# Six explicit drains of GpSimd in a fused attention, MLP and routed-expert kernel: one beside the MLP, one in each unrolled block of the expert loop

## The chip, the cores and the metric

The kernel runs on one core of one Trainium2 chip. The metric is the device time of one execution in microseconds (us), lower is better. It is given as the median of several executions. Engines are named as the profile names them: PE (TensorE matmul), PEld (its weight load), DVE (VectorE), ACT (ScalarE), POOL (GpSimd), SP (SyncE). A "q" behind a name (POOLq) is the engine's sequencer: waits, branches, register work, drains. L12 is line 12 of the kernel before.

## What is computed

A linear-attention recurrence over 4 batches, 8 heads, 768 tokens, head width 48, then an MLP (384 to 2048 to 384, leaky with slope 0.01), then a routed layer: each of the 3072 tokens whose skip score is positive goes through one of 8 experts.

```python
cur = einsum('bhd,bhe->bhde', u * kt, vt)
y[t] = einsum('bhd,bhde->bhe', rt, state + cur)
state = w * state + einsum('bhd,bhe->bhde', kt, vt)
...
h = x @ w_in; z = maximum(0.01 * h, h) @ w_out
...
chosen = (z @ w_skip) > 0; e = argmax(z[chosen] @ w_gate)
h = maximum(zc @ w1[e], 0); y = gate_w * (h @ w2[e])
out = z; out[chosen] = zc + y
```

## The kernel before

Matrix products are done in split float32 (three products of high and low parts), so PE carries nearly the whole span. The program has two stages.

**Attention and MLP.** 24 chunks of 128 tokens form 8 groups of 3 chunks (GROUPS = 8, CPG = 3). While PE works on the MLP of a group, the attention of the next group runs between its steps. When the MLP of a group is done, DVE picks the expert of each token and computes a spot (`dst`). POOL then writes token numbers and gate weights to `id_list` in DRAM with three indirect DMAs per group (`scatter(G)`, L1927): 7 groups (LATE = 7) before the last one, whose turn comes after two early gathers.

**Experts.** Blocks of 128 token rows are handled by expert. Two blocks "ahead" have their own code (`gather_ahead` L1950, `scatter_ahead` L1956). The others are in a loop that is unrolled by four (UNROLL = 4); this input runs it over 12 blocks. For block j, POOL's part is `put_rows(j, u, turn)`:

- it waits until the rows of block j-1 have landed in `out` (L2005, the wait shows on L2006 together with the increment of `s_res_free`, which lets DVE reuse a result buffer),
- it copies the row numbers of block j to `put` (L2007), and, while block j+4 exists, those of block j+4 to `get` (L1978),
- it waits for DVE's result (`s_res_done`, L2014, which shows on L2015), scatters the rows to `out` (L2016), and, while block j+4 exists, gathers its rows (`gather`, L1983).

All of POOL's DMAs are indirect ones whose descriptors GpSimd itself writes. There is no other kind of order at work: each engine runs its instructions as they are written. After the loop POOL waits for all rows to have landed (L2032, which shows on the branch of L100), and then every engine drains and meets the others at the barrier that closes the block of engine programs; all of that has line L100 (`nc.Block()`'s exit). The program that is put ahead of the kernel (L2074) has a drain on each engine too.

Of the kernel before, what the change touches and what calls it, by code (L numbers as in the profile page):

```python
# [92 lines left out]
def build(nc, rk_t, rk_nat, v_nat, w_cols, u_rows, win, wout, wout_t, gates, experts, consts, out, z_rows):  # L93
# [6 lines left out]
    with ctx:  # L100
# [555 lines left out]
        def _(pe):  # L656
# [347 lines left out]
            with pe.Fori(0, (BLOCKS + 1) // UNROLL) as jj:  # L1004
                with pe.If(UNROLL * jj < blocks):
                    for u in range(UNROLL):
                        j = UNROLL * jj + u
                        with pe.If(j < blocks):
                            cur, odd, _, _, nxt, nxt_odd = entries(pe, regs, j)
                            with pe.If(j < blocks - 1):  # L1010
                                pe.wait_ge(s_zt_lo, j + 2)
                                pe.wait_ge(s_w1_lo, PIECES * nxt + PIECES)
                                first_product((u + 1) % 2, nxt_odd * EW)

                            with pe.If(j < blocks - 2):
                                pe.wait_ge(rows_in[(u + 2) % UNROLL], 16 * (jj + 1 + (u + 2) // UNROLL))
                                turn_rows((u + 2) % UNROLL)

                            if u == 1:
                                pe.wait_ge(s_res_a, AHEAD)  # L1020
                            pe.wait_ge(s_eht_lo, 2 * j + 1)
                            pe.wait_ge(s_w2_lo, PIECES * cur + PIECES)
                            second_product(u % 2, odd * EW, 0)
                            pe.wait_ge(s_eht_lo, 2 * j + 2)
                            with pe.If(j < blocks - 1):
                                pe.wait_ge(s_relu_done, j + 2)
                                turn_hidden()
                            second_product(u % 2, odd * EW, 1)
# [3 lines left out]
        def _(act):  # L1032
# [282 lines left out]
            with act.Fori(0, (BLOCKS + 1) // UNROLL) as jj:  # L1315
                with act.If(UNROLL * jj < blocks):
                    for u in range(UNROLL):
                        j = UNROLL * jj + u
                        with act.If(j < blocks):
                            e, odd, new, _, e_next, odd_next, new_next, _ = entries(act, regs, j)  # L1320
                            for half in range(2):
                                act.wait_ge(s_eht_done, 2 * j + half + 1)
# [578 lines left out]
        def _(pool):  # L1901
# [18 lines left out]
            def scatter(G):  # L1920

                if G == 0:
                    pool.wait_ge(s_zero_out, 32)
                pool.wait_ge(s_dst, 2 * (G + 1))
                for i in range(CPG):
                    n = CPG * G + i
                    pool.indirect_dma_start(  # L1927
                        out=id_list[:, :], out_offset=bass.IndirectOffsetOnAxis(ap=dst[:, n:n + 1], axis=0),
                        in_=idgate[:, n, :], in_offset=None, bounds_check=P * SPOTS - 1,
                        oob_is_err=False).then_inc(s_scatter, 16)  # L1930
# [29 lines left out]

            for G in range(LATE):
                scatter(G)
            pool.wait_ge(s_set, 16 * CPG)
            pool.wait_ge(s_z_store, 16 * 2 * KNOWN)
            pool.wait_ge(s_order, 2)
# [6 lines left out]
            def spot_at(reg, j):  # L1972

                pool.load(reg, plan[0:1, bass.ds(FIELDS * j + SPOT, 1)])
                return pool.snap(reg, min_val=0, max_val=SPOTS - 1)

            def pick_ids(u, spot_j):
                pool.tensor_copy(get[u][:], id_get[:, bass.ds(spot_j, 1)]).then_inc(s_ids_get, 1)  # L1978

            def gather(u, j):  # L1980
                pool.wait_ge(s_ids_get, j + 1)
                pool.sem_inc(s_pool_past, 1)
                pool.indirect_dma_start(  # L1983
                    out=zg[u][:], out_offset=None, in_=z_rows[:, :],
                    in_offset=bass.IndirectOffsetOnAxis(ap=get[u][:, 0:1], axis=0)).then_inc(rows_in[u], 16)
# [18 lines left out]
            def put_rows(j, u, turn):  # L2004
                pool.wait_ge(s_rows_out, 16 * (j + AHEAD))  # L2005
                pool.sem_inc(s_res_free, 1)  # L2006
                pool.tensor_copy(put[u % 2][:], id_put[:, bass.ds(spot_at(reg, j), 1)]).then_inc(s_ids_put, 1)  # L2007
                pool.wait_ge(s_ids_put, j + 1)
                pool.sem_inc(s_pool_past, 1)
                with pool.If(j < blocks - UNROLL):  # L2010
                    pool.wait_ge(rows_in[u], 16 * (turn + 1))
                    pool.sem_inc(s_pool_past, 1)
                    pick_ids(u, spot_at(far, j + UNROLL))
                pool.wait_ge(s_res_done, j + 1)  # L2014
                pool.sem_inc(s_pool_past, 1)  # L2015
                pool.indirect_dma_start(  # L2016
                    out=out[:, :], out_offset=bass.IndirectOffsetOnAxis(ap=put[u % 2][:, 0:1], axis=0),
                    in_=res[u % 2][:], in_offset=None, bounds_check=TOKENS - 1,
                    oob_is_err=False).then_inc(s_rows_out, 16)
                with pool.If(j < blocks - UNROLL):  # L2020
                    gather(u, j + UNROLL)

            turns = (BLOCKS + 1) // UNROLL
            with pool.Fori(0, 2) as part:
                with pool.If(turns // 2 * UNROLL * part < blocks):
                    with pool.Fori(0, turns // 2) as jj:
                        with pool.If(turns // 2 * UNROLL * part + UNROLL * jj < blocks):
                            for u in range(UNROLL):
                                j = turns // 2 * UNROLL * part + UNROLL * jj + u
                                with pool.If(j < blocks):  # L2030
                                    put_rows(j, u, turns // 2 * part + jj)
# [51 lines left out]
```

## Time and profile before

| | us |
|---|---|
| median of 3 runs | 669.46 (668.72 to 670.49) |
| profiled execution, its own time | 666.72 |
| span of that execution | 665.0 |
| PE busy | 646.2 (97%) |
| POOL busy | 86.0 (13%) |
| mean granted TensorE clock | 0.996 |

The span is the time from the first to the last instruction that the profiler saw; the execution's own time is 1.7 us more. POOL's busy time counts its copies and the writing of descriptors, not its sequencer's work and not drains.

### The profile page before, as it was taken

The page shows a single profiled execution, that of the slowest core. Times are in us where ns is not written, and L with a number is a line of the kernel's source. Part 1 is how long each engine was busy: PE and PEld are TensorE (multiplying, and loading weights), DVE is VectorE, ACT ScalarE, POOL GpSimd, SP SyncE. Part 2 cuts the span into 40 slices and gives each one's busy share as a digit, 9 for nine tenths or more (in the row PEclk, how much of TensorE's full clock was granted, in tenths as well). Part 3 has the DMA queues.
Part 4 walks back from the last instruction along what each step waited for, and adds up shares of the span by engine and source line. Part 5 has one row for each costly group of instructions (what it writes and reads, how often), then busy time and mean ns, then how long its engine had stood idle before and what let it go on. Part 6 is the DMA issues. An engine that isn't in the chain of part 4 may idle for free.

```text
span 665.0 us, 14201 instructions
## 1 busy us (share of the span) xinstructions
PE 646.2 (97%) x4733; PEld 606.9 (91%) x4734; DVE 401.4 (60%) x867; ACT 309.5 (47%) x683; POOL 86.0 (13%) x102
## 2 busy tenths in 40 slices
PE   8989999999999999999999999999999989999994
PEld 7878999999999999999999999999999879989993
DVE  7876765656656575466555545653466854865752
ACT  5466534345334443454434344333346435746650
POOL 5240000100010001001000100010021141423311
PEclk9999999999999999999999999999999999999998
DMA  8935625220422321242114221201505267686300
GB/s 226 301 130 205 212 72 174 73 71 18 134 68 71 96 75 54 64 143 73 48 30 139 73 72 30 76 8 57 213 1 206 92 199 277 207 284 264 130 21 8
DMA packets 39325, 78.09 MB, mean 117 GB/s; under 512 B 9032, under 2 KB 27494, under 8 KB 39216
## 3 DMA queue, kind: packets, MB, share of 16 engines
q1 hardware_dynamic: 34272, 62.96, 30.2%
q10 hardware_dynamic: 2432, 9.76, 4.3%
q0 software_dynamic: 2560, 4.58, 2.2%
q8 instruction: 36, 0.59, 0.4%
q14 instruction: 25, 0.20, 0.1%
HBM read 61.68 MB, written 13.00 MB: 112 GB/s over the span
## 4 chain that ended last, share of the span: by engine, by line
PE 89%; DVE 3%; ACT 2%; issue 2%; DMA 1%; POOL 1%; SPq 0%; ACTq 0%; POOLq 0%; DVEq 0%
PE bank L808 31%; PE bank L831 30%; PE bank L908 8%; PE bank L925 7%; PE bank L673 3%; PE bank L735 3%; PE bank L742 2%; PE bank L756 1%; PE bank L916 1%; DMA stage<-in_rk_t 1%; PE bank L865 1%; PE bank L901 1%; ACT am L1100 1%; PE bank L716 0%; DMA zg<-z_rows,get 0%
## 5 line engine op out<-in xcount | busy, mean ns | idle before, releaser
L1138 ACT ACTIVATE h_sb<-bank 128x384 f32<-128x384 f32 x128 | 62.8, 491 | 221.6 <-PE bank L808 221.4
L1448 DVE TENSOR_TENSOR h_sb<-h_sb,bank 128x384 f32<-128x384 f32 x128 | 70.9, 554 | 156.2 <-ACT h_sb L1138 156.2
L808 PE MATMUL bank<-x_hi,win_hi 128*128 128x384 f32 x384 | 135.1, 352 | 1.0 <-DVE win_lo L1494 0.6
L831 PE MATMUL bank<-wout_hi,g_hi 128*128 128x394 f32 x384 | 132.0, 344 | 0.4 <-DVE state L1424 0.4
L831 PE MATMUL bank<-wout_hi,g_lo 128*128 128x394 f32 x384 | 131.2, 342 | 0.0
L831 PE MATMUL bank<-wout_lo,g_hi 128*128 128x394 f32 x384 | 131.1, 342 | 0.0
L808 PE MATMUL bank<-x_hi,win_lo 128*128 128x384 f32 x384 | 129.5, 337 | 0.0
L808 PE MATMUL bank<-x_lo,win_hi 128*128 128x384 f32 x384 | 129.3, 337 | 0.0
L1455 DVE TENSOR_TENSOR g_lo<-h_sb,g_hi 128x384 fp32r<-128x384 f32 x128 | 71.8, 561 | 30.7 <-ACT g_hi L1145 29.7
L1145 ACT ACTIVATE g_hi<-h_sb 128x384 fp32r<-128x384 f32 x128 | 66.7, 521 | 42.3 <-DVE h_sb L1448 40.9
L1927 POOL DMA_INDIRECT id_list<-idgate,dst x24 | 24.4, 1016 | 449.0 <-DVE dst L1655 444.1
L808 PEld LDWEIGHTS bank<-x_hi,win_hi 128*128 128x128 f32 x384 | 72.1, 188 | 8.4 <-issue 5.8
L831 PEld LDWEIGHTS bank<-wout_hi,g_hi 128*128 128x128 f32 x384 | 72.2, 188 | 0.7 <-issue 0.7
L831 PEld LDWEIGHTS bank<-wout_hi,g_lo 128*128 128x128 f32 x384 | 72.3, 188 | 0.0
L831 PEld LDWEIGHTS bank<-wout_lo,g_hi 128*128 128x128 f32 x384 | 72.3, 188 | 0.0
L808 PEld LDWEIGHTS bank<-x_lo,win_hi 128*128 128x128 f32 x384 | 72.3, 188 | 0.0
L808 PEld LDWEIGHTS bank<-x_hi,win_lo 128*128 128x128 f32 x384 | 72.1, 188 | 0.0
L1100 ACT ACTIVATE am<-const,diag 128x128 f32<-128x128 f32 x184 | 58.1, 392 | 2.4 <-DVE wout_lo L1508 2.3
L925 PE MATMUL bank<-w_hi,eht_hi 128*128 x96 | 34.1, 356 | 0.6 <-DVE eht_lo L1851 0.6
L1411 DVE COPY_PREDICATED am<-const,bank 128x512 f32<-128x512 uint32 x46 | 31.3, 737 | 3.0 <-ACT am L1100 2.9
L925 PE MATMUL bank<-w_hi,eht_lo 128*128 x96 | 32.3, 337 | 0.0
L925 PE MATMUL bank<-w_lo,eht_hi 128*128 x96 | 32.3, 336 | 0.0
(250 smaller groups left out, 895.5 us busy)
## 6 DMA issues: line engine op xcount, KB each, us to landing
raw<-in_experts SPq DMA_DIRECT2D x32, 768.0 KB, 6.0
rkt<-in_rk_t SPq DMA_DIRECT2D x46, 192.0 KB, 3.7
rkn<-in_rk_nat SPq DMA_DIRECT2D x21, 384.0 KB, 4.4
v<-in_v_nat SPq DMA_DIRECT2D x24, 192.0 KB, 3.0
z_rows<-z_sb SPq DMA_DIRECT2D x24, 192.0 KB, 2.8
out<-z_sb SPq DMA_DIRECT2D x24, 192.0 KB, 2.8
stage<-in_win ACTq DMA_DIRECT2D x4, 768.0 KB, 4.5
stage<-in_wout_t ACTq DMA_DIRECT2D x4, 768.0 KB, 6.6
```

The source lines that it names most:

```text
L673: mm = pe.matmul(scores_in(n)[q][:, P * p:P * p + P], kb[n % 2][rows, p, :], rt[n % 2][rows, p, :], start=True, stop=True)
L808: mm = pe.matmul(h_ps[t % 2][:, 0:GT], a[:, kk, cols], b[G % 2][:, kk, :], start=n == 0, stop=n == 3 * KT - 1)
L831: mm = pe.matmul(z_ps[i][:, 0:ZW], a[t % 3][:, tok], b[:, f, :], start=f == 0 and j == 0, stop=f == FT - 1 and j == 2)
L908: mm = pe.matmul(eh_ps[c][:], a[par][:, kk, :], b[:, bass.ds(base + EF * kk + 512 * c, 512)], start=kk == 0 and a is zt_hi and b is w1_hi, ...
L925: mm = pe.matmul(ey_ps[par][:, 0:DM], a[:, f, :], b[:, bass.ds(base + DM * f, DM)], start=f == 0 and a is hi and b is w2_hi, stop=f == EFT ...
L1100: ins = act.activation(am_of(n)[h % 2][:, h // 2, :], ident, ACT.Copy, scale=diag_of(n)[:, h:h + 1])
L1138: act.activation(h_sb[t % 2][:], h_ps[t % 2][:, 0:GT], ACT.Copy, scale=SLOPE).then_inc(s_h_scaled, 1)
L1145: act.activation(g_hi[t % 3][:], h_sb[t % 2][:], ACT.Copy).then_inc(s_g_hi_done, 1)
L1411: dve.copy_predicated(am_of(n)[q][:], spread(before.bitcast(U32), 1, [P, PAIRS, P]), scores_in(n)[q][:].rearrange("a (p t) -> a p t", p=PA ...
L1448: dve.tensor_tensor(h_sb[t % 2][:], h_sb[t % 2][:], h_ps[t % 2][:, 0:GT], ALU.max).then_inc(s_leaky, 1)
L1455: dve.tensor_tensor(g_lo[t % 3][:], h_sb[t % 2][:], g_hi[t % 3][:].bitcast(F32), ALU.subtract).then_inc(s_g_lo_done, 1)
L1927: pool.indirect_dma_start(out=id_list[:, :], out_offset=bass.IndirectOffsetOnAxis(ap=dst[:, n:n + 1], axis=0), in_=idgate[:, n, :], in_off ...
```

## The change

One `pool.drain()` stands behind the scatters of the seven groups, ahead of the waits for the two early gathers. Another stands in `put_rows`, behind the wait for the rows of the block before and the increment of `s_res_free`, ahead of the copy to `put`. As `put_rows` is unrolled four times, the second one is in the program four times and runs 12 times here. Nothing else is changed, moved or taken away; no other engine's program differs.

```diff
@@ -1960,6 +1960,7 @@
 
             for G in range(LATE):
                 scatter(G)
+            pool.drain()
             pool.wait_ge(s_set, 16 * CPG)
             pool.wait_ge(s_z_store, 16 * 2 * KNOWN)
             pool.wait_ge(s_order, 2)
@@ -2004,6 +2005,7 @@
             def put_rows(j, u, turn):
                 pool.wait_ge(s_rows_out, 16 * (j + AHEAD))
                 pool.sem_inc(s_res_free, 1)
+                pool.drain()
                 pool.tensor_copy(put[u % 2][:], id_put[:, bass.ds(spot_at(reg, j), 1)]).then_inc(s_ids_put, 1)
                 pool.wait_ge(s_ids_put, j + 1)
                 pool.sem_inc(s_pool_past, 1)
```

## Rows read from the trace of the kernel before

**Rows 1.** The page: the span of the profiled execution.
```profile
span 665.0 us, 14201 instructions
```

**Rows 2.** The chain that ended last, 655 to 666 us: start, us, what.
```profile
656.26 0.63 DVE res L1895
...
657.83 0.93 POOL out L2016
```

**Rows 3.** Line L100, the closing barrier: count, duration ns min/median/max, starts.
```profile
L100 SPq DRAIN  x1: 7/7/7, 629.2 to 629.2; - x1
...
L100 DVEq DRAIN  x1: 17/17/17, 660.2 to 660.2; - x1
L100 POOLq COMPARE_BRANCH  x1: 38/38/38, 660.3 to 660.3; - x1
L100 POOLq DRAIN  x1: 4324/4324/4324, 660.4 to 660.4; - x1
```

**Rows 4.** Line L2074, the program's start, the same columns.
```profile
L2074 POOLq DRAIN  x1: 188/188/188, 0.4 to 0.4; - x1
...
L2074 POOL MEMSET const-uint8-127<- x1: 118/118/118, 0.4 to 0.4; 128x1 uint8 x1
```

**Rows 5.** Groups of instructions of POOL: count, busy us, mean ns, idle before.
```profile
L1927 POOL DMA_INDIRECT id_list<-idgate,dst x24 | 24.4, 1016 | 449.0 <-DVE dst L1655 444.1 <-issue 4.9
L1983 POOL DMA_INDIRECT zg<-z_rows,get x12 | 15.0, 1247 | 5.7 <-POOL get L1978 3.3 <-issue 2.4
L2016 POOL DMA_INDIRECT out<-res,put x12 | 14.9, 1245 | 36.6 <-DVE res L1895 25.7 <-issue 9.6 <-POOL get L1978 1.4
...
L1956 POOL DMA_INDIRECT out<-zg_a,put_a x2 | 3.0, 1498 | 2.6 <-DVE zg_a L1563 2.3 <-issue 0.3
L1950 POOL DMA_INDIRECT zg_a<-z_rows,get_a x2 | 2.9, 1460 | 6.9 <-DVE put_a L1534 6.6 <-issue 0.3
```

**Rows 6.** POOL in order of time, around the place of the first drain.
```profile
492.77 1.73 POOL L1927 DMA_INDIRECT id_list<-idgate,dst  x1 [0.30 <-issue]
501.11 0.98 POOL L1950 DMA_INDIRECT zg_a<-z_rows,get_a  x1 [6.61 <-DVE put_a L1534]
```

**Rows 7.** POOL in order of time, blocks 0, 4 and 5 of the loop.
```profile
553.80 0.18 POOL L2007 COPY put<-id_put 128x1 uint32 x1 [7.79 <-DMA out<-zg_a,put_a]
...
557.33 0.99 POOL L2016 DMA_INDIRECT out<-res,put  x1 [2.10 <-DVE res L1895]
...
594.73 0.18 POOL L2007 COPY put<-id_put 128x1 uint32 x1 [4.36 <-DMA out<-res,put]
...
596.84 1.01 POOL L2016 DMA_INDIRECT out<-res,put  x1 [0.69 <-POOL get L1978]
...
603.67 0.18 POOL L2007 COPY put<-id_put 128x1 uint32 x1 [4.54 <-DMA out<-res,put]
```

**Rows 8.** POOL in order of time, the last block.
```profile
656.40 0.18 POOL L2007 COPY put<-id_put 128x1 uint32 x1 [1.86 <-DMA out<-res,put]
657.79 0.98 POOL L2016 DMA_INDIRECT out<-res,put  x1 [1.20 <-DVE res L1895]
```

**Rows 9.** Lines L2006, L2010 and L2015 from 652 us on: POOL's sequencer.
```profile
L2006 POOLq EVENT_SEMAPHORE  x1: 17/17/17, 655.8 to 655.8; - x1
...
L2010 POOLq COMPARE_BRANCH  x1: 45/45/45, 656.8 to 656.8; - x1
...
L2015 POOLq EVENT_SEMAPHORE  x2: 17/17/17, 652.6 to 656.9; - x2
```

**Rows 10.** The chain that ended last, two blocks of the loop.
```profile
594.25 4.13 PE bank L908 x18
...
603.75 4.13 PE bank L908 x18
```

**Rows 11.** The page's DMA issues: count, KB each, median us to landing.
```profile
zg<-z_rows,get POOLq DMA_INDIRECT x12, 4.8
out<-res,put POOLq DMA_INDIRECT x12, 3.7
```

## The prediction

> **What bounds the kernel now.** I read the page first, then the chain of work that ended last, then what stands behind that chain's end. Of a span of 665.0 us [rows 1], PE is busy for 97% and POOL for 13% (the table above). So through most of the span a change on POOL costs or gives nothing, unless it makes another engine late. The chain of the last microseconds [rows 2] goes from DVE's last result (656.26 us, 0.63 long) to POOL's last scatter, which starts at 657.83 us by that view and has written its descriptors by 658.8. The span ends at 665.0. The view does not cover these last 6.2 us, and they belong to POOL alone: its sequencer passes the last wait (all rows landed) at 660.3 us, then a DRAIN starts at 660.4 and takes 4,324 ns [rows 3]. DVE's own closing drain, the latest of the other engines', is at 660.2 us and takes 17 ns; SP's took 7 ns [rows 3]. So the last 4.3 us of the kernel are one drain on POOL, with nothing beside it, and every engine waits for it at the barrier. That is the part of the profile that this change can touch.
>
> **What a drain on POOL costs.** The trace holds two. The one at the program's start takes 188 ns, while POOL finishes its fourth small MEMSET of 118 ns [rows 4]; it started about when the MEMSET did, so it held on for at most some 0.07 us of its own. The one at the end takes 4,324 ns, and it has no instruction of POOL to wait for: the last descriptors were written 1.6 us earlier [rows 8], and the wait ahead of it says that their rows have landed. Between the two drains POOL issued 24 + 12 + 12 + 2 + 2 = 52 indirect DMAs [rows 5], and never drained. Hence my reading: a drain on POOL clears up after each DMA issued since the last drain. One costs (4.324 - 0.188) / 52 = 0.080 us to 4.324 / 52 = 0.083 us. The fixed part is between 0 and 0.19 us. The bounds for any one of the added drains are 7 ns (the drain of SP) and 4,324 ns (the final one); I take the value per DMA, since two prices that differ by a factor of 23 need something that grew between them.
>
> **The change part by part.**
> The drain beside the MLP clears 21 DMAs: 0.19 + 21 x 0.08 = 1.9 us. It starts when the last of these has its descriptors, 492.77 + 1.73 = 494.5 us, and POOL's next work is at 501.11 us, held by DVE's `put_a` [rows 6]. Of these 6.6 us idle it takes 1.9: hidden, cost nothing. Were it 4.3 us long it would still fit.
> The drain of block 0 clears the 2 early gathers, 3 late scatters, 4 gathers and 2 scatters ahead: 11 DMAs, 0.9 + 0.19 = 1.1 us. POOL's copy in that block is at 553.80 us, and ahead of its scatter at 557.33 POOL stood idle for 2.10 us, until DVE's result was there [rows 7], so it is hidden.
> Blocks 1 to 11 clear one scatter and, up to block 8, one gather: 2 x 0.08 plus up to 0.19, so 0.2 to 0.35 us. The increment that frees DVE's buffer stands ahead of the drain, so DVE isn't held. Queued behind the drain are the copies, the scatter and the gather of four blocks on. In blocks like 4, POOL itself is the last to be ready: copy at 594.73, scatter at 596.84, held by POOL's own `get` copy [rows 7]. There the scatter goes out 0.3 us later. Nobody notices: PE takes 9.5 us for a block (594.25 to 603.75) [rows 10], whereas POOL's own round is 0.6 us from the wait to the copy (655.8 to 656.4) [rows 8, 9], 2.1 us from the copy to the scatter [rows 7], and 3.7 us to the landing [rows 11], 6.4 us in all. Even the slow round from 594.73 to 603.67 is 8.9 us [rows 7], and a delay there is made good in a block with a faster landing. A gather is issued two blocks ahead of the transposes that need it.
> The last block is on the path. POOL passes the head at 655.8, its branch of L2010 ends at 656.8 and its wait for DVE's result is met at 656.9 us [rows 9]: 0.1 us of slack. The added drain clears one scatter, 0.08 plus 0.05 to 0.19, and costs its own issue of about 0.05: 0.2 to 0.3 us, of which 0.1 is covered. Loss: 0.1 to 0.2 us.
> The closing drain has one scatter left to clear instead of 52: 0.13 to 0.27 us in place of 4.32. Gain: 4.05 to 4.2 us.
> Sum: 4.1 - 0.15 = 4.0 us, nearly all of it behind the last scatter. On the profiled execution's own time that is 666.72 - 4.0 = 662.7 us. That execution was 2.7 us below the median of the runs shown; by the same ratio (0.9940) the median goes from 669.46 to 665.5 us.
>
> **A rule weighed against a row.** At the start and the end of the program the drains of SP and DVE took 7 to 17 ns, but the two of POOL 188 and 4,324 ns [rows 3, 4]. The Trainium skill ("VectorE: DVE Perf Modes", section "The DRAIN you can't avoid") says of the drains of the preamble and postamble that they are a constant of about 12 ns on all five engines. The trace agrees for SP and DVE and differs for POOL. By that rule the 13 executed drains would cost nothing and the closing one would have nothing to give: 669.5 us, the second rival below.
>
> **The rivals.**
> *Each drain behind a DMA costs a fixed 4.3 us* (asking all queues whether they are idle, say), however few DMAs stand behind it. For it: the start drain stood behind no DMA at all, so two prices fit this as well as mine. Against it: nothing in the trace but the wish for a cause. It decides in the last block and at the end: with a fixed cost f the change gives 4.3 + 0.1 - 2f, so it is level at f = 2.2 us, faster by less than 0.3% above 1.2 and slower by over 0.3% from 3.2. At 4.3 the loop is bound by POOL as well: the round of 6.4 us becomes 10.7, longer than PE's 9.5. From the first head, 0.6 us ahead of the copy at 553.8 us, 12 such rounds last to 681.6; less about 0.8 for each of the last four blocks, which have no second copy, 678.4; the closing drain and barrier add 4.8. The span is then 683 to 686 us, that is +20, and the median about 690 us. Chance 0.12.
> *The 4.3 us belong to the kernel's end and not to DMAs since the last drain* (something that only the closing sequence has to wait for). Then the added drains are short ones of 0.2 us, hidden but for 0.1 us in the last block, and the time stays at 669.5 us. For it: the one long drain is also the one at the end. Against it: all rows had landed when it began, and the other engines passed their drains in 7 to 17 ns [rows 3]. Chance 0.12.
> *Part fixed, part per DMA*, f between 0.3 and 1.2 us: gain 2.0 to 3.8 us, 665.7 to 667.5 us. Chance 0.07; f from 1.2 to 2.2, no measurable change, 0.03.
> *A drain also waits for transfers in flight.* At the heads of blocks 1 to 8 the gather of the block before may be under way: issued 1.3 us behind the scatter, with 4.8 against 3.7 us to landing [rows 11], it lands 2.4 us later. POOL's round is then 8.8 us, still below 9.5, and from block 9 on there is no gather. The time is my forecast's, and this is counted in it.
>
> **How the numbers follow.** My forecast has 0.66. The runs of before differ by 0.15% to either side, so what can be told from no change is about 0.3%, 2.0 us. Faster by more than that: 0.66 + 0.07 = 0.73. Same: 0.12 + 0.03 = 0.15. Slower: 0.12. The likeliest case has its own range, 664.3 to 667.0 us: 4.2 us of gain and a median 0.7 below, or 3.3 of gain and one 0.8 above. The range for 8 in 10 takes in no change as well: 664.0 to 670.2 us. The fixed cost of 4.3 us lies outside of it.
>
> **What would show it.** Right: the closing DRAIN of POOL is 0.1 to 0.3 us in place of 4.32, the one beside the MLP is about 1.9 us long (21 DMAs), block 0's about 1.1 (11 DMAs) and the others 0.1 to 0.4; the last scatter, which now starts 0.9 us behind the end of DVE's last result (656.89 to 657.79) [rows 2, 8], starts 1.0 to 1.1 us behind it; PE's rounds stay at 9.5 us. Wrong: a drain with one or two DMAs behind it that takes over a microsecond, or a closing drain that is still long. A drain in the middle of the loop that is far longer than that of the last block, with the closing one short, would mean that it waits for transfers in flight, or is held by DVE; it changes no number above as long as POOL's round stays below PE's.

## The result

| | before | after |
|---|---|---|
| median of 8 runs each | 668.73 us (667.11 to 670.49) | 663.97 us (662.86 to 666.79) |
| span of the profiled execution | 665.0 us | 662.7 us |
| closing drain of POOL | 4.324 us | 0.128 us |
| from the start of DVE's last result to the span's end | 8.7 us | 4.5 us |

The ratio is 0.9933, with a 95% interval of 0.9916 to 0.995: 4.5 us faster (3.3 to 5.6). In a later session the same kernel gave 0.9944 (0.9925 to 0.9962). The prediction of 4.0 us less holds. Its time of 665.5 us was worked out from a median before of 669.46 us, where the eight runs have 668.73; by the measured ratio that median becomes 665.0. As a plain time the 663.97 us measured lies 0.3 us below the likeliest range (664.3 to 667.0) and at the very edge of the range for 8 in 10 (664.0 to 670.2). And of the six drains in the title only five are in the program, one and four; they run 13 times.

The closing lines of the kernel after, with count, duration in ns (min/median/max) and starts, answer to [rows 3]:

```profile
L100 DVEq DRAIN  x1: 17/17/17, 662.1 to 662.1; - x1
L100 POOLq COMPARE_BRANCH  x1: 38/38/38, 662.2 to 662.2; - x1
L100 POOLq DRAIN  x1: 128/128/128, 662.4 to 662.4; - x1
```

The last wait is passed at 662.2 us and the drain behind it is now 128 ns long. DVE's closing drain stands at 662.1 us, 0.3 us ahead of POOL's, so little more could be had from POOL before DVE held the barrier.

The added drains of the kernel after, one beside the MLP (L1963) and some of the twelve in the loop (L2008, one query for each place), the same columns:

```profile
L1963 POOLq DRAIN  x1: 5462/5462/5462, 492.9 to 492.9; - x1
...
L2008 POOLq DRAIN  x1: 970/970/970, 553.9 to 553.9; - x1
...
L2008 POOLq DRAIN  x1: 552/552/552, 583.5 to 583.5; - x1
...
L2008 POOLq DRAIN  x1: 5198/5198/5198, 612.5 to 612.5; - x1
...
L2008 POOLq DRAIN  x1: 134/134/134, 642.1 to 642.1; - x1
L2008 POOLq DRAIN  x1: 118/118/118, 648.0 to 648.0; - x1
L2008 POOLq DRAIN  x1: 125/125/125, 657.6 to 657.6; - x1
```

POOL in order of time around the first and the last of them (start, us, idle time before in brackets), and DVE's last result:

```profile
494.65 1.74 POOL L1927 DMA_INDIRECT id_list<-idgate,dst  x1 [0.30 <-issue]
502.99 0.98 POOL L1950 DMA_INDIRECT zg_a<-z_rows,get_a  x1 [6.61 <-DVE put_a L1534]
...
598.69 1.01 POOL L2018 DMA_INDIRECT out<-res,put  x1 [1.25 <-DVE res L1895]
...
609.22 1.52 POOL L2018 DMA_INDIRECT out<-res,put  x1 [0.46 <-POOL get L1979]
...
621.82 1.01 POOL L2018 DMA_INDIRECT out<-res,put  x1 [0.15 <-POOL get L1979]
...
658.17 0.62 DVE L1895 SCALAR_TENSOR_TENSOR res<-bank,found,zg 128x384 f32<-128x384 f32 x1 [3.73 <-PE bank L925]
659.72 0.98 POOL L2018 DMA_INDIRECT out<-res,put  x1 [1.20 <-DVE res L1895]
```

A drain's row starts when the sequencer comes to it, not when POOL has nothing else to do. The drain of L1963 starts at 492.9 us, but the last scatter ahead of it has its descriptors only at 494.65 + 1.74 = 496.39. It ends at 498.4, so its own part is 2.0 us, with 21 DMAs to clear. The wait behind it is as long as before, 6.61 us, held by the same instruction: hidden whole.

Why the two spans differ by 2.3 us only, when the closing drain is 4.2 shorter: the scatter of group 6 that starts at 492.77 us in [rows 6] starts at 494.65 here, 1.9 us later, ahead of any added drain. The very first of these scatters is as late already (125.15 us before, 127.14 after). The stretch of 0 to 150 us tells why (elapsed, busy us of PE, PEld, DVE, ACT and POOL, granted clock, DMA share, GB/s), first before, then after:

```profile
0.00:150.00 150.00, 143.89 (x1319) 132.60 (x1321) 101.81 (x223) 76.47 (x186) 22.75 (x29) 1.00 0.54 162
```

```profile
0.00:150.00 150.00, 143.37 (x1308) 132.06 (x1310) 101.07 (x221) 75.70 (x184) 23.26 (x29) 0.99 0.55 162
```

PE was granted 0.99 of its clock there and not 1.00: from 14.7 to 18.1 us the granted clock was 0.50 (the level of 1.2 GHz) in this execution and 1.00 (2.4 GHz) in the one before; in the 7.0 us ahead of it PE was busy for 5.73 us, before for 6.31. No added drain has run by then, and the change doesn't decide it: 0.98 came up for a kernel with one drain, 1.00 for another with several. So single executions are best compared from an event behind the MLP, and I use the start of DVE's last result.

### The profile page after: what moved, and what is told of

It is laid out like the page before. It is cut to its first block, busy times and chain, and to the rows that moved or that the text cites. A ratio compares the mean times of both kernels' runs of the same rounds, so it can differ in the third digit from the quotient of the medians.

```text
span 662.7 us, 14214 instructions
## 1 busy us (share of the span) xinstructions
PE 647.7 (98%) x4733; PEld 608.1 (92%) x4734; DVE 401.4 (61%) x867; ACT 310.1 (47%) x683; POOL 87.0 (13%) x102
## 3 DMA queue, kind: packets, MB, share of 16 engines
q0 software_dynamic: 2560, 4.58, 2.1%
## 4 chain that ended last, share of the span: by engine, by line
PE 88%; DVE 4%; issue 2%; ACT 2%; DMA 2%; POOL 1%; SPq 0%; ACTq 0%; POOLq 0%; DVEq 0%
PE bank L808 31%; PE bank L831 30%; PE bank L908 8%; PE bank L925 6%; PE bank L673 4%; PE bank L735 3%; PE bank L742 2%; PE bank L756 1%; PE bank L916 1%; DMA stage<-in_rk_t 1%; ACT am L1100 1%; PE bank L901 1%; PE bank L716 1%; DMA zg<-z_rows,get 0%; DVE w_lo L1548 0%
```

## The experiments

Twelve runs follow: nine kernels, and two of these and the changed kernel once more. Line numbers in their rows are their own. "Tail" is the time from the start of DVE's last result to the end of the span in the profiled execution.

| kernel | DMAs that the closing drain has to clear | closing drain, us | tail, us | ratio to before (95%) |
|---|---|---|---|---|
| before | 52 | 4.324 | 8.7 | 1 |
| changed kernel | 1 | 0.128 | 4.5 | 0.9933 (0.9916 to 0.995) |
| mlp_only | 31 | 2.606 | 7.0 | 0.9969 (0.9944 to 0.9993) |
| loop_only | 1 | 0.128 | 4.6 | 0.9951 (0.9923 to 0.998) |
| end_only | 0 | 0.034 | 7.9 | 0.9996 (0.9978 to 1.0015) |
| more_full | 73 | 6.039 | 10.4 | one run, 673.56 us |
| more_few | 73 | 6.039 | 10.4 | one run, 674.18 us |
| double_drain | 1 | 0.128 | 4.6 | one run, 663.46 us |
| foot | 0 | 0.060 | 6.4 | 1.0001 (0.9976 to 1.0025) |
| once_in_four | 3 | 0.294 | 4.6 | 0.9921 (0.9892 to 0.9951) |
| foot_again | 0 | 0.060 | 6.4 | 0.999 (0.9974 to 1.0007) |
| foot_late | 0 | 0.055 | 6.4 | 0.9978 (0.9965 to 0.999) |
| after_again | 1 | 0.128 | 4.5 | 0.9944 (0.9925 to 0.9962) |
| once_again | 3 | 0.294 | 4.6 | 0.9946 (0.9927 to 0.9964) |

**mlp_only.** The drain beside the MLP alone.

```diff
             for G in range(LATE):
                 scatter(G)
+            pool.drain()
```

> Only the drain beside the MLP. By the theory that a drain clears 0.083 us per indirect DMA since the last drain, the MLP's drain ends 2.0 us behind its last descriptors (in the changed kernel 492.9 + 5.46 = 498.4 against 494.65 + 1.74 = 496.4) and the closing drain has 31 of 52 DMAs left: 31 x 0.083 + 0.04 = 2.6 us, a gain of 1.7 us. By the rival that a drain grows with the time since the last one (4.324 us in 660 us), the closing drain, 165 us behind the MLP's, takes 1.1 us, a gain of 3.2 us.

The closing drain of this kernel:

```profile
L100 POOLq DRAIN  x1: 2606/2606/2606, 662.8 to 662.8; - x1
```

2.606 us for 31 DMAs, as worked out per DMA; the price by elapsed time (1.1 us) falls. The tail is 1.7 us shorter than before, and the ratio is worth 2.1 us (0.5 to 3.7).

**loop_only.** The drains in the loop alone.

```diff
                 pool.sem_inc(s_res_free, 1)
+                pool.drain()
```

> Only the drains at the heads of the blocks. Per DMA: block 0's drain has 32 DMAs to clear, 2.7 us (the changed kernel's took 0.97 for 11), the closing one 0.13 us, and the whole gain of the change, 4 us, is here already, since the drain of block 0 fits into POOL's idle time of 2.1 us ahead of its scatter but for some tenths. By time since the last drain: block 0's drain takes 553 x 4.324 / 660 = 3.6 us.

Its first drain in the loop, at the head of block 0:

```profile
L2007 POOLq DRAIN  x1: 2688/2688/2688, 554.0 to 554.0; - x1
```

2.688 us for 32 DMAs, 0.082 more than mlp_only's closing one with 31. Nothing of it is seen at the end: the tail is 4.6 us, within 0.1 of the changed kernel's. So the drain beside the MLP gives nothing once the ones in the loop are there.

**end_only.** One drain, behind the last scatter.

```diff
+            pool.drain()
             pool.wait_ge(s_rows_out, 16 * (blocks + AHEAD))
```

> One drain, behind the last scatter and ahead of the final wait for the rows. It has 52 DMAs to clear, the last of them in flight. If a drain clears finished DMAs while it waits for the one in flight, it starts 1.0 us earlier than the closing drain of before (loop left at 659.3, closing drain at 660.4) and the kernel gains 0.9 us, with a closing drain of 0.05. If it waits for all transfers first and clears then, it ends where the closing drain of before ended, and the gain is 0 (-0.1 to 0.1).

The added drain and the closing one of this kernel:

```profile
L2032 POOLq DRAIN  x1: 4324/4324/4324, 659.2 to 659.2; - x1
```

```profile
L100 POOLq COMPARE_BRANCH  x1: 43/43/43, 663.6 to 663.6; - x1
L100 POOLq DRAIN  x1: 34/34/34, 663.8 to 663.8; - x1
```

The drain has the same 4,324 ns as before, although it starts with a scatter in flight (issued at 657.63, landed 2.4 us later, at 660.0). It clears finished DMAs beside that landing, so it ends earlier by as much as it starts earlier, 1.1 us counted from DVE's last result. The final wait and the second drain behind it take 0.3 us back: tail 7.9 against 8.7 us, 0.8 of the 0.9 expected. By the times of the runs it is no more than level with before (0.9996, whose interval holds the expected 0.9987).

**more_full and more_few.** No drain added, 21 DMAs added: every scatter beside the MLP once more, with all rows or with 16.

```diff
                         oob_is_err=False).then_inc(s_scatter, 16)
+                if G < LATE:
+                    pool.wait_ge(s_scatter, 16 * CPG * (G + 1))
+                    for i in range(CPG):
+                        n = CPG * G + i
+                        pool.indirect_dma_start(
+                            out=id_list[:, :], out_offset=bass.IndirectOffsetOnAxis(ap=dst[0:128, n:n + 1], axis=0),
+                            in_=idgate[0:128, n, :], in_offset=None, bounds_check=P * SPOTS - 1,
+                            oob_is_err=False).then_inc(s_again, 16)
...
             sp.wait_ge(s_scatter, 16 * KNOWN)
+            sp.wait_ge(s_again, 16 * KNOWN)
```

more_few has 16 in place of the two 128.

> No added drain; each of the 21 scatters beside the MLP is issued a second time, with the same 128 rows, behind a wait for the first. 73 DMAs stand behind the closing drain. Per DMA (and per row as well): 73 x 0.083 = 6.1 us, the kernel 1.75 us slower. By time since the last drain, or fixed: 4.3 us as before, no slower.

> As the kernel with 21 scatters issued twice, but the second time with 16 of the 128 rows. If the price is per DMA: closing drain 6.1 us. If it is per row or descriptor: 21 x 16 / 128 = 2.6 DMAs' worth more, 4.5 us.

The closing drains of the first and the second kernel:

```profile
L100 POOLq DRAIN  x1: 6039/6039/6039, 665.5 to 665.5; - x1
```

```profile
L100 POOLq DRAIN  x1: 6039/6039/6039, 666.2 to 666.2; - x1
```

Equal to the nanosecond: the price does not go by rows, not by time, and it is not fixed. By themselves the two kernels don't separate a price per DMA from one per packet, since the DMA queue of GpSimd shows the same number of packets in both, 32 for each added scatter (packets, MB, share; 2560 packets before):

```profile
q0 software_dynamic: 3232, 4.60, 2.3%
```

```profile
q0 software_dynamic: 3232, 4.58, 2.2%
```

The other drains settle that. A block's scatter has 64 packets, and clearing one costs the same 0.082 us (the closing 0.128 us of the changed kernel, less the fixed part measured in double_drain below). So the price is per DMA.

Both kernels were slower by 5.6 and 6.1 us in their one run. Of this the tail shows 1.7 us, the growth of the drain: 10.4 us against 8.7. The rest lies ahead of DVE's last result, where the second scatters put off what POOL does behind the MLP (its first early gather starts at 507.66 and 508.63 us, before at 501.11) and the clock was below that of before (0.993 and 0.990 against 0.996).

**double_drain.** The changed kernel with each drain of the loop written twice.

```diff
                 pool.drain()
+                pool.drain()
```

> The changed kernel with the drain at each block's head written twice. The second one has nothing to clear and nothing in flight behind the first, so it shows the fixed part alone: 0.04 to 0.06 us by the theory per DMA (0.118 to 0.134 us with one DMA, less 0.083), against 0.188 or more if a drain has a large fixed part. The time is that of the changed kernel, 0.1 us more in the last block.

The second ones:

```profile
L2009 POOLq DRAIN  x12: 46/46/53, 554.1 to 656.7; - x12
```

A drain with nothing to clear takes 0.046 us here; as a closing drain it took 0.034 in end_only and 0.060 in foot. With the longer ones this is a line. N DMAs cost 0.046 + 0.082 N us: 0.294 for 3 gives 0.083 each, 0.970 for 11 gives 0.084, 2.606 for 31 gives 0.083, 4.324 for 52 gives 0.082, 6.039 for 73 gives 0.082.

**once_in_four.** Only the second of the four unrolled blocks drains.

```diff
-                pool.drain()
+                if u == 1:
+                    pool.drain()
```

> The drain beside the MLP stays, and of the loop's four copies only the second has one, so blocks 1, 5 and 9 drain. The closing drain has the scatters of blocks 9 to 11 left, 3 DMAs: 0.29 us in place of 0.13; the last block has no drain of its own, 0.0 to 0.15 us less. Time as the changed kernel, within 0.2 us: ratio to before 0.993 to 0.995. The rival that the drains in the loop cost something by holding POOL up to 5 us would make it faster than the changed kernel by more than that.

Measured: closing drain 0.294 us for 3 DMAs, tail 4.6 us, ratio 0.9921. The scatter of the last block starts 1.50 us behind DVE's result (656.46 to 657.96), as in mlp_only (1.50), end_only and before (1.52 and 1.53), against 1.55 in the changed kernel, 1.58 in loop_only and 1.64 in double_drain. Against the 1.50 us without a drain, one in the last block costs the path 0.05 to 0.08 us, two of them 0.14.

**foot.** The loop's drain stands behind the block's DMAs and not ahead of them.

```diff
                 with pool.If(j < blocks - UNROLL):
                     gather(u, j + UNROLL)
+                pool.drain()
```

> The drain beside the MLP stays; the one of the loop stands at the foot of a block, behind its scatter and gather, instead of the head. If a drain waits for transfers in flight, each of the first 8 ends some 0.15 us behind the landing of the gather, 4 to 8 us behind its issue, and the last block's ends behind the landing of the last scatter (2.2 us), so that the exit of the loop, 1.3 us, no longer lies beside that landing: gain against before 3.0 us, 1.0 less than the changed kernel, with a closing drain of 0.05. If it does not wait for transfers, all are 0.2 us behind the last descriptors and the gain is 4.0 us.

All twelve of them, and the last one alone:

```profile
L2023 POOLq DRAIN  x12: 2338/4842/8398, 558.3 to 658.4; - x12
```

```profile
L2023 POOLq DRAIN  x1: 2582/2582/2582, 658.4 to 658.4; - x1
```

A drain does wait for transfers in flight. The last scatter was issued at 658.5 and landed 2.4 us later, at 660.9; the drain ended at 661.0. In the middle of the loop the gather's landing makes them up to 8.4 us long: the longest ended at 616.35 us, 0.13 behind the landing of its gather. The tail is 6.4 us: 1.9 longer than with the drain at the head, where I had expected 1.0. The loop's exit (expected 1.3 us) took 1.7, and the last block's head came late by the drain of the block before. The runs, however, were level with before (1.0001), where a tail 2.3 us shorter should give 0.9966. That expectation missed, and I measured it again.

**foot_again, foot_late, after_again, once_again.** Four kernels on one chip. foot_late drains at the foot only where no gather is in flight:

```diff
-                pool.drain()
+                with pool.If(j > blocks - UNROLL - 1):
+                    pool.drain()
```

> The kernel with the drain at the foot of each block, once more beside the others on one chip. Its profiled execution ended 4.6 us behind the start of its last scatter, against 7.2 before, with PE's rounds at 9.5 us, yet its runs were level with before. By the theory that only the end counts, the ratio is 0.996 (2.5 us less), and the first measurement was the spread between executions. By the rival that holding POOL 5 to 8 us in each block makes PE late in some executions, it is 1.000 again.

> The drain at the foot of a block only in the last four blocks, which have no gather. The end is that of the kernel with a drain at each foot plus a branch of 0.1 to 0.2 us: ratio 0.9965 by both theories. If it is clearly below that of the kernel with the drain at each foot, holding POOL in the middle of the loop costs time.

> The changed kernel as it is, beside the others: ratio 0.9933 to 0.9945 (4.0 us less by the sum of the prediction, 4.1 by the closing drain of 0.13 us).

> The kernel that drains in one of four blocks, beside the others. By the drains' lengths it is level with the changed kernel within 0.2 us (0.0003 of the ratio). If holding POOL costs time in some executions, it is faster than the changed kernel, by half a microsecond or more.

foot_again came out at 0.999 (0.9974 to 1.0007), again not at 0.9966. foot_late has the same tail (6.4 us) and 0.9978 (0.9965 to 0.999), whose lower end just holds the expected 0.9965. The two intervals overlap, so that the waits in the middle of the loop cost time at the foot is likely and not shown. The changed kernel and the one that drains once in four are level, 0.9944 and 0.9946. So the long waits inside the changed kernel's loop cost nothing that these runs can tell (half a microsecond could hide in intervals of 1.2 us to either side), whereas longer ones, at the foot, seem to cost some 2 us of the median: 2.3 in the first session, 1.7 in the second.

## Why the prediction held, step by step

**What bounds the end.** Right. The last 4.3 us were POOL's drain, and taking it away took 4.2 us off the tail (8.7 to 4.5).

**The price of a drain.** Right, and the experiments show what was inferred from two rows. I had 0.080 to 0.083 us per DMA and a fixed part of 0 to 0.19; measured are 0.082 and 0.046. The fixed 4.3 us, the first rival, falls with a drain of 46 ns. The second, that the 4.3 us belong to the kernel's end, falls with end_only, where the added drain took the 4,324 ns and the closing one 34. The third, part fixed and part per DMA, falls by the same line.

**The rule set against it.** A constant of some 12 ns for every engine's closing drain (the Trainium skill, "VectorE: DVE Perf Modes", section "The DRAIN you can't avoid") is near what the other engines show here, 7 to 17 ns in both kernels, and does not hold for a POOL that has issued DMAs. That section speaks of the drains of preamble and postamble; that it takes in this closing one was the prediction's reading.

**Beside the MLP.** 1.9 us worked out, 2.0 us measured behind its last descriptors, hidden as said. The line of double_drain gives 1.8 for 21 DMAs; the 0.2 above it are not explained. By loop_only it isn't needed.

**Block 0.** 1.1 us worked out, 0.970 measured, hidden.

**Blocks 1 to 8.** Here the size was off. The sum had 0.2 to 0.35 us each; they took 0.46 to 5.2. Six of the eight took over a microsecond with two DMAs behind them, which the prediction names as a sign of being wrong; its last sentence gives the reason that turned out true. The step that was mis-sized is the fourth rival's, the wait for a transfer in flight, which I put at 2.4 us from median landing times. The gather issued in block 2, at 580.3 us, landed 3.7 us later, at 584.0, and the drain of block 3, of 583.5 us, ended at 584.05. The gather issued in block 5, at 611.05, had the loads of the experts' weights beside it (197 GB/s in all from 610 to 620 us) and landed at 617.5, and the drain of block 6 lasted until 617.65. POOL's rounds there were not below PE's 9.5 us, as I had made a condition: 598.69 to 609.22 is 10.5 us and on to 621.82 is 12.6, and both of those scatters were held by POOL's own copies. PE lost nothing. Its rounds, from the chain that ended last of the kernel after:

```profile
605.69 4.12 PE bank L908 x18
...
615.18 4.13 PE bank L908 x18
...
624.69 4.13 PE bank L908 x18
...
634.23 4.13 PE bank L908 x18
```

These stay at 9.5 us, and the ten rounds from 547.62 to 643.73 us take 96.1, against 96.0 before (545.85 to 641.83). The condition was too strict: DVE waits for the head of the block before, where `s_res_free` is raised ahead of the drain, and PE needs a gather's rows only some time after they have landed. The scatter of block 6 starts 6.5 us behind DVE's result (615.35 to 621.82), before 1.6 (613.46 to 615.08); in block 9 it is 1.5 again, since from there on there is no gather and the drains take 0.118 to 0.134 us.

How near PE came to being late is seen where it loads the rows that the gather issued in block 6 has fetched (L901). After, and then before:

```profile
L1984 POOL DMA_INDIRECT zg<-z_rows,get x1: 1155/1155/1155, 623.1 to 623.1; - x1
...
DMA to landing us min/median/max: 4.5/4.5/4.5
...
L901 PEld LDWEIGHTS bank<-const,zg x3: 138/142/143, 628.4 to 628.8; 128*128 128x128 f32 x3
```

```profile
L1983 POOL DMA_INDIRECT zg<-z_rows,get x1: 1937/1937/1937, 616.4 to 616.4; - x1
...
DMA to landing us min/median/max: 4.8/4.8/4.8
...
L901 PEld LDWEIGHTS bank<-const,zg x3: 138/142/142, 626.5 to 626.9; 128*128 128x128 f32 x3
```

The rows are there 0.7 us ahead of their use, where it was 5.4 before (whose own closest gather, the one issued in block 2, has 1.0), and in after_again it is 0.4. "Two blocks ahead", as the prediction has it, is right by the count of PE's blocks, but in time the gather is issued 5.3 us ahead (10.1 before). So the time came out although the stated condition did not hold, by a margin that the prediction had not worked out: in part luck.

**The last block.** 0.1 to 0.2 us of loss worked out, of which the runs show less. The scatter starts 1.55 us behind the start of DVE's result; before it was 1.53 (656.26 to 657.79), and 1.50 in the kernels where POOL was ready first. The loss is 0.02 us against before and 0.05 against those kernels. From the end of DVE's result it is 0.93 us to the scatter, where the prediction's sign was 1.0 to 1.1.

**The closing drain.** 0.13 to 0.27 us worked out, 0.128 measured.

**The range.** 4.2 us of gain and a median 0.7 below give 664.6 us, not the 664.3 that the prediction has as the lower end of its likeliest range; both are above the 663.97 measured.

**Open.** Why the drain at the foot of each block gives none of its 2.3 us in the first session's runs and 0.6 in the second's. Its two profiled executions were of the shorter ones (664.93 us with a median of 668.06, and 664.97 with 666.85), and PE's rounds in them are 9.5 us, so no trace shows the place. That POOL, held up to 8.4 us, makes PE late in the other executions is argued, not shown. For it: in both traces the rows of the same gather land only 0.6 us ahead of their use, in foot_late 5.3. Against it: the changed kernel's margin is as thin and its runs show no loss. The mean granted clock doesn't tell the executions apart either: foot_again has 664.33 and 668.32 us, both at 0.998.

## What to carry to other kernels

Look behind the last row of the chain of work: a closing drain of GpSimd costs 0.05 us plus 0.08 us for each indirect DMA that it issued since its last drain, with everything else already done. Drain where GpSimd is idle and has nothing in flight, late enough that few DMAs follow. Four drains in the run, one beside the MLP and three in the loop, were as good here as thirteen; a single one in the loop was not tried. Don't put a drain right behind a DMA, since it waits until that has landed, and look at how long before its use each transfer lands that is issued behind the drain.

## What was not expected of the hardware

The price of clearing does not depend on the size of a DMA: 21 scatters of 16 rows and 21 of 128 rows lengthened the drain by the same 1.715 us, 0.082 each, and a scatter with 64 packets in place of 32 costs that too. A drain clears finished DMAs while another one is in flight: 4,324 ns with a scatter under way, 4,324 ns without. And with the clock granted to PE in the first 150 us (0.98 to 1.00) the first scatter beside the MLP moved from 125.15 us (before) to 129.26 us (after_again), 4.1 us, which is as much as the change itself gives.
